# Loading and splitting the last stage's first weights in the first two expert blocks instead of in attention

## What is computed

```python
# 1. attention: (2, 8, 768, 64), window of 16 and the maxima/means of 24 blocks
a = softmax(concat([scores_local_masked, scores_block_summaries]))
x = (a @ concat([v, v_block_mean])).reshape(1536, 512)
# 2. 8 experts, top 1: w1 (8, 512, 1024), w2 (8, 1024, 512)
out[mask] = gate_w[mask, None] * (np.maximum(x[mask] @ w1[e], 0.0) @ w2[e])
# 3. dense: w_in (512, 2048), w_out (2048, 512)
h = np.maximum(x @ w_in, 0.0)
out = h * h @ w_out
```

## Time and profile before

| | us |
|---|---|
| median of 3 runs | 599.38 |
| lowest, highest run | 595.86, 601.61 |
| the profiled execution's span | 599.6 |
| TensorE busy in it | 578.1 |
| VectorE, ScalarE, POOL busy | 285.5, 251.2, 95.7 |

### The profile page before, as it was taken

How to read it: one execution, slowest core, us unless ns; L and a number is a source line. 1 busy time by engine, 2 the same in 40 slices (tenths; PEclk the granted TensorE clock), 3 DMA queues, 4 the chain that set the end, 5 groups by cost and what they waited for, 6 DMA issues and landing times.

```text
span 599.6 us, 11061 instructions
## 1 busy us (share of the span) xinstructions
PE 578.1 (96%) x4259; PEld 506.3 (84%) x4259; DVE 285.5 (48%) x422; ACT 251.2 (42%) x517; POOL 95.7 (16%) x125
## 2 busy tenths in 40 slices
PE   7898999999999999999999999999999999999997
PEld 6776776599899898898888989889899998988986
DVE  5989886565556465475563223223323323222321
ACT  4788886824445544354452123222222212222221
POOL 7467850031022021130210000000000000000000
PEclk9789889989999999999999999999999999999999
DMA  7967896058676494684711002002001001000000
GB/s 223 262 201 209 227 188 181 27 176 303 233 272 224 149 317 134 226 281 147 271 62 44 1 1 72 0 1 70 0 0 70 0 0 69 1 0 36 1 0 36
DMA packets 66044, 70.68 MB, mean 118 GB/s; under 512 B 25784, under 2 KB 50360, under 8 KB 65632
## 3 DMA queue, kind: packets, MB, share of 16 engines
q1 hardware_dynamic: 62400, 58.17, 32.0%
q0 software_dynamic: 3616, 12.13, 5.8%
HBM read 60.22 MB, written 10.06 MB: 117 GB/s over the span
## 4 chain that ended last, share of the span: by engine, by line
PE 63%; issue 12%; DMA 11%; POOL 6%; DVE 4%; ACT 1%; SPq 1%; POOLq 1%; ACTq 0%; DVEq 0%
PE psum L799 19%; PE psum L801 19%; PE psum L800 19%; DMA x_rows_sb<-x_rows,idx_g 5%; DMA win_raw<-in_moe_w_in 3%; PE psum L592 3%; POOL win_lo L495 2%; DVE wa_lo L1340 2%; PE psum L793 1%; POOL win_hi L493 1%; DMA v_blk<-in_v 1%; ACT wa_hi L1019 1%; POOL v_blk L506 1%; PE psum L852 1%; DMA q_raw<-in_q 1%
## 5 line engine op out<-in xcount | busy, mean ns | idle before, releaser
L799 PE MATMUL psum<-x_hi,win_hi 128*128 128x256 f32 x384 | 108.4, 282 | 1.2 <-DVE x_lo L1388 1.2
L801 PE MATMUL psum<-x_hi,win_lo 128*128 128x256 f32 x384 | 108.4, 282 | 0.0
L800 PE MATMUL psum<-x_lo,win_hi 128*128 128x256 f32 x384 | 108.2, 282 | 0.0
L1398 DVE TENSOR_TENSOR h_sq<-h_relu 128x512 f32<-128x512 f32 x48 | 33.3, 694 | 133.4 <-ACT h_relu L1073 133.4
L1073 ACT ACTIVATE h_relu<-psum 128x512 f32<-128x512 f32 x48 | 28.7, 599 | 134.6 <-PE psum L801 134.6
L799 PE MATMUL psum<-wb_hi,h_hi 128*128 128x512 f32 x208 | 83.4, 401 | 0.0
L800 PE MATMUL psum<-wb_lo,h_hi 128*128 128x512 f32 x208 | 82.3, 396 | 0.0
L801 PE MATMUL psum<-wb_hi,h_lo 128*128 128x512 f32 x208 | 82.2, 395 | 0.0
L799 PEld LDWEIGHTS psum<-x_hi,win_hi 128*128 128x128 f32 x384 | 73.3, 191 | 2.9 <-issue 1.4
L800 PEld LDWEIGHTS psum<-x_lo,win_hi 128*128 128x128 f32 x384 | 73.3, 191 | 1.7
L801 PEld LDWEIGHTS psum<-x_hi,win_lo 128*128 128x128 f32 x384 | 73.3, 191 | 0.0
(11 more groups left out here) (184 smaller groups left out, 998.0 us busy)
## 6 DMA issues: line engine op xcount, KB each, us to landing
w_raw<-in_moe_w SPq DMA_DIRECT2D x56, 512.0 KB, 3.9
win_raw<-in_moe_w_in POOLq DMA_DIRECT2D x8, 512.0 KB, 5.8
w_raw<-in_moe_w_out SPq DMA_DIRECT2D x8, 512.0 KB, 4.0
k_raw<-in_k SPq DMA_DIRECT2D x8, 384.0 KB, 5.1
q_raw<-in_q SPq DMA_DIRECT2D x8, 384.0 KB, 5.0
v_blk<-in_v SPq DMA_DIRECT2D x3, 1024.0 KB, 6.0
v_win<-in_v SPq DMA_DIRECT2D x16, 192.0 KB
x_rows<-x_all SPq DMA_DIRECT2D x8, 384.0 KB, 4.7
```

The lines of the kernel that those rows point to most:

```text
L799: pe.matmul(o, l_hi, r_hi, start=start, stop=False)
L800: pe.matmul(o, l_hi, r_lo, start=False, stop=False)
L801: return pe.matmul(o, l_lo, r_hi, start=False, stop=stop)
L1398: dve.tensor_tensor(h_sq[c % 2][:, :], h_relu[c % 2][:, :], h_relu[c % 2][:, :], ALU.mult)\
```

## The change

The eight loads and splits of `w_in` leave their place behind POOL's constants. Two loads and splits 0 to 3 now stand between gather(1) and scatter(0), splits 4 to 7 between gather(2) and scatter(1); the loop over the blocks starts at 2. Each split but the last two is followed by the load of the piece after next. The buffers `win_raw` get a place in memory of their own, three tiles of attention move within memory, and SP's wait for the splits ahead of the first expert weights goes. The instructions that are issued stay the same; the splits are written out instead of looped.

```diff
+        win_raw = [sb(f"win_raw{i}", [P, PIECE]) for i in range(2)]
...
-        win_raw = [sb(f"win_raw{i}", [P, PIECE], scope=one) for i in range(2)]
...
             sp.wait_ge(blocks_made, 1)
-            sp.wait_ge(win_split, PAIRS2)
...
-            load_win(0, 0)
-            load_win(1, 1)
-            with pool.Fori(0, PAIRS2 // 2 - 1) as it:
-                for par in range(2):
-                    split_win(it, par)
-            for par in range(2):
-                split_win(PAIRS2 // 2 - 1, par, ahead=False)
...
             gather(0, first=True)
             pool.wait_ge(routed, 1)
             gather(1)
+            load_win(0, 0)
+            load_win(1, 1)
+            for pair in range(PAIRS2 // 2):
+                split_win(pair)
             scatter(0, first=True)
-            with pool.Fori(1, nblk) as b:
+            gather(2)
+            for pair in range(PAIRS2 // 2, PAIRS2):
+                split_win(pair, ahead=pair + 2 < PAIRS2)
+            scatter(1)
+            with pool.Fori(2, nblk) as b:
                 gather(b + 1)
                 scatter(b)
```

More of the change, by code:

```diff
@@ L114, in build @@
         prob_t = sb("prob_t", [COLS, 2, GT * P], scope=one)
-        win_raw = [sb(f"win_raw{i}", [P, PIECE], scope=one) for i in range(2)]
+        emb_sb = sb("emb_sb", [E, DM], scope=one)
+        emb_n = sb("emb_n", [E, DM], scope=one)
+        sq_e = sb("sq_e", [E, DM], scope=one)
         tri = sb("tri", [P, P], scope=one)
@@ L127, in build @@
         before = sb("before", [NT * E, NT, E], scope=one)
-        emb_sb = sb("emb_sb", [E, DM], scope=one)
-        emb_n = sb("emb_n", [E, DM], scope=one)
         emb_t = sb("emb_t", [P, KC, E], scope=one)
-        sq_e = sb("sq_e", [E, DM], scope=one)
         nrm_e = sb("nrm_e", [E, 8], scope=one)
@@ L484, in load_win, with split_win @@
                     .then_inc(win_loaded[par], 16)
-            def split_win(it, par, ahead=True):
-                pair = 2 * it + par
-                pool.wait_ge(win_loaded[par], 16 * (it + 1))
+            def split_win(pair, ahead=True):
+                par = pair % 2
+                pool.wait_ge(win_loaded[par], 16 * (pair // 2 + 1))
                 end_waits()
-                hi = win_hi[:, bass.ds(pair * PIECE, PIECE)]
-                lo = win_lo[:, bass.ds(pair * PIECE, PIECE)]
+                hi = win_hi[:, pair * PIECE:(pair + 1) * PIECE]
+                lo = win_lo[:, pair * PIECE:(pair + 1) * PIECE]
                 pool.tensor_copy(hi, win_raw[par][:, :]).then_inc(win_hi_made, 1)
@@ L552, in gather @@
                     pool.tensor_copy(idx_g[:, :], gather_tab[:, bass.ds(2 * b, 2)]).then_inc(idx_made, 1)
-                    pool.wait_ge(idx_made, 1 if isinstance(b, int) else 2 * b - 2)
+                    pool.wait_ge(idx_made, max(1, 2 * b - 2) if isinstance(b, int) else 2 * b - 2)
                     end_waits()
```

## The result

The changed kernel takes 612.38 us (median of 4 runs, 610.67 to 619.37) against 598.97 us (4 runs, 595.86 to 601.61): a ratio of 1.0227, 95% interval 1.0173 to 1.0281. It is slower, by 13 us; the forecast was 603 and its range ended at 609. A later set of runs on another occasion gave 613.24 against 601.42 us, 1.0198 (1.0168 to 1.0227).

The account below looks back on a forecast made before the run. TensorE, busy 578.1 of 599.6 us, bounds the kernel, so changes come from its gaps and low clock. Terms -4 + 4.6 + 1.5 + 1.5 = +3.6 on 599.6 gave 603 us, range 595 to 609.

Parts of the forecast that it names:

- A: Whole kernel: the forecast's own sum of gains and stalls holds, 600 to 606 us; chance 0.5.
- C: Expert blocks: loads land after 9 us, DVE holds up each of eight splits once, 608 to 613 us; chance 0.2.
- Attention: Attention, 37 to 88 us: removing eight loads and splits ends DVE's waits for POOL, -4 us (0 to -6.7).
- The floor: Attention's first three head-pair steps: they shrink to ScalarE's 9.5 us plus about 0.2 for handoffs, 9.7 each.
- SP's wait and the layout: Ahead of the expert weights: removing SP's wait for the splits and moving tiles in memory changes nothing, 0 us.
- Splits 0 to 3: Between gather(1) and scatter(0): loads and splits delay POOL's scatters and TensorE's start on the gathered rows, +4.6 us.
- The clock: Expert blocks, behind TensorE's gap of nearly 5 us: work runs at a lower granted clock, +1.5 us (0 to 1.7).
- Splits 4 to 7: Between gather(2) and scatter(1): the splits and DVE's subtracts delay gather(3), +1.5 us (0 to 4).
- The last stage's wait: Last stage: its wait for the splits costs 0, since the last four are done in the second of seven blocks.
- The base: Whole kernel: all changes count against the profiled execution's span of 599.6 us, 0.2 over the median of 599.4.
- B: Expert blocks: the new place hides the splits, loads landing in under 5 us, 593.9 to 596.6 us; chance 0.2.
- D: Attention: gives nothing back since ScalarE is busy 9.5 of each 10.7 us, 607.2 us; chance 0.1.

Follow-up runs that it names:

- the port by itself: Kernel with two splits a block and gathers ahead of scatters, plus eight splits' casts and subtracts on a zeroed tile in attention, no loads: 596.24 us, ratio 0.9975.
- loads alone, in denser order: Kernel with two splits ahead of each scatter, plus eight unused w_in loads in attention, issued back to back: 602.82 us, ratio 1.0073.
- this half alone: Changed kernel with splits 0 to 3 back in attention, 4 to 7 still behind gather(2): 604.44 us, ratio 1.0106.

## Why the prediction was wrong, point by point

The mechanism was the right one: the gathers behind the splits in POOL's queue, two waits of TensorE at the named turns of rows, a low clock behind the first, and the old period of 24 us afterwards. The sizes were not, and the forecast chose A where C came. By its steps, in the profiled executions:

1. *Attention*: -4 forecast, -6.0 measured, within its bounds; 0.9 of it is luck ahead of POOL's first load, which leaves 5.1. The floor was well placed (9.7 us a step forecast; 10.3, 9.7, 9.5 measured). Under-sized was the fourth step: from its start (78.76 before, 74.80 after) to the next masked scores it took 9.8 us before and 6.9 after, where I gave 1.1. The cause was right in the main: the port by itself costs 4.0 to 4.7 us. "The 4 MB less of transfers removes no wait that I can find" left out one wait of 0.4 us, and loads alone, in denser order, cost 8 to 9 us between the same marks, so traffic can cost more than this sentence lets expect. How the 5.1 of this change divide isn't shown.
2. *SP's wait and the layout*: 0 forecast, 0.7 to 4 us by the interval, a profile like that of before. Held but for some 1 us.
3. *Splits 0 to 3*: +4.6 forecast, +9.2 measured. This is the step that failed first. Four parts came out longer: the landing at 9.4 instead of 7 (+2.4); one reload also late (+2.5), which the sum didn't have at all, as it took POOL for busy all the time; the port 2.3 us over three instructions instead of 1.2 (+1.1), and 0.4 more around each split (+1.5). Against them the gather landed only some 3.5 us after its issue and not 6 (-2.5): the DMA engines' share fell from 0.92 to 0.36 while it was under way, where it was 1.03 before. gather(1)'s second issue was 0.6 us shorter than before, which leaves the 4.6 that were missing.
4. *The clock*: +1.5 forecast. The work of 176.1 to 180.1 and 207.7 to 210.6 us ran at half speed, which makes 2.0 and 1.4 us; the second gap had been left out, being forecast too small for it. By runs only the second is shown (1.3 us). The first lies ahead of the wait for gather(3), whose time POOL's queue set, so without it that wait would probably have been longer by as much: not tested.
5. *Splits 4 to 7*: +1.5 forecast, a wait of 6.0 measured, and 6.55 with this half alone. From the end of gather(2)'s issues to the end of gather(3)'s POOL needed 24.0 us before, 29.1 in the changed kernel and 29.8 with this half alone. The splits ended 18.7 us behind gather(2), near the 18 of the forecast. What was missed stands behind them: POOL's copies of indices took 1.20 and 0.90 us instead of 0.2, the second scatter started 22.4 us behind gather(2) and not 20.3, and the gather(3) issues took 1.7 us each instead of 1.0, all beside DVE's subtracts. With this half alone that is nearly the whole wait. In the changed kernel two more things stand against each other. TensorE's need of gather(3) counts from when it begins on gather(2)'s rows, and that was 5.2 us after POOL's issue before and 2.6 here, because the late gather landed sooner (+2.6); and its work up to turn 3 took 1.9 us longer at the low clock (-1.9 of wait).
6. *The last stage's wait*: 0, held.
7. *The base.* I set the span of 599.6 equal to the time. A run's time is 1.6 to 1.9 us above its span in both kernels, so the profiled execution before was one of about 601.4, at the slow end of its runs (the median is 598.97). The two slips cancel: 599.4 + 3.6 is the 603 that I gave, as a median. That is luck, and no part of the miss.

The sum of 9.7 us in spans: -7.7 by turn 1, +9.2, +7.7 (6.0 of wait, the rest the clock), +1.1, -0.5. The remaining difference to the medians' 13.4 is that of the executions profiled: the median before lies 2.4 us below the profiled execution, that of the changed kernel 1.3 above its own (611.07).

Of the rivals, C (late loads and the port both ways, 608 to 613) is what came: the first scatter went out at 167.87, 175.6 on the old scale and so behind C's 172, though only five of the casts and subtracts were held up by DVE, and not each of the eight splits. B's condition, a first split before 147 us, failed (it started at 143.25 with everything 7.7 us early, so 150.9 on the old scale). Its "no low clock behind so short a gap" had no ground either: attention's clock had fallen behind waits for the copy of no more than 1.3 us. D fell: ScalarE's floor did not keep attention from shrinking.

## What to carry to other kernels

An engine that is idle for long is not free: look at what stands behind the new work in its queue, and how much slack the first consumer of that has. Here an idle time of 16 us took two splits a block for a wait of 0.8 us, and four in each of two blocks made 15 us of stalls. If work must go into such a queue, put it in portions below the slack, and the issue that others wait for ahead of it. And when a chain has several terms of which each can only be late, don't take the middle of each: landing, reload and port all came out on the late side together. That full DMA engines and a busy DVE made them late together is likely; it wasn't tested.

## What the runs showed of the hardware that was not expected

- *POOL's cast and subtract wait for DVE's subtracts* too, not only DVE for POOL's: 1.04 to 2.04 us and 2.35 to 3.28 us, 0.4 to 1.0 us more each time. Four DVE subtracts took 8.16 us instead of 4.63. Both sides pay.
- *POOL's issue of an indirect transfer waits for such DVE work*: 1.73 and 1.74 us instead of 0.96 to 1.0, for gather(3) at 198.78 and 200.81 us. DVE's subtracts there, of the changed kernel:

```profile
198.43 1.21 DVE L1326 TENSOR_TENSOR wb_lo<-w_raw,wb_hi 128x1024 fp32r<-128x1024 f32 x1
...
200.48 1.23 DVE L1326 TENSOR_TENSOR wb_lo<-w_raw,wb_hi 128x1024 fp32r<-128x1024 f32 x1 [0.24 <-ACT wb_hi L1005]
```

  Both issues began inside a subtract and ended 0.87 and 0.84 us behind its end. The kernel before has it too: the issue at 140.48 took 1.57 us, 0.81 of them behind the end of a subtract. In twelve of the profiles, from 120 to 320 us, every indirect issue of over 1.07 us began while DVE's `wa_lo` or `wb_lo` subtracts were running.
- *The landing of the same 512 KB load* ranged from 3.7 to 10.4 us in the expert blocks of the changed kernel.
- *The spread of whole runs goes with the mean granted clock*: the four runs of the changed kernel with mean granted clock 0.978, 0.978, 0.968 and 0.960 took 610.67, 611.07, 613.70 and 619.37 us.
